# The last stage's products of a fused attention and two-layer MLP chain: seven block products for eight

## The reference, cut to what matters

```
attn_out = linear attention with decay, x = [3072, 512]
x = mixture of 8 experts over x (top 1), again [3072, 512]
a = x @ w1            # [3072, 1024]
b = x @ w2            # [3072, 1024]
out = ((a * b) @ w3) @ w_out     # [3072, 512]
```

## Time and profile before

| | us |
|---|---|
| median of 3 runs | 878.25 |
| lowest and highest | 874.43, 881.44 |
| profiled execution | 881.25 |
| its span, first to last instruction | 879.5 |
| TensorE busy | 855.1 |
| VectorE busy | 283.7 |
| ScalarE busy | 236.2 |
| GpSimd busy | 89.5 |
| mean granted clock of TensorE | 0.987 |

### The profile page before, as it was taken

The page is one execution under the profiler, slowest core; times in us unless marked ns, Lnnn a source line. Parts: engine busy times, 40 slices in busy tenths (PEclk is TensorE's granted clock), DMA queues, the critical chain, the costliest instruction groups (busy, mean ns, idle before and its releaser), DMA issues.

```text
span 879.5 us, 14619 instructions
## 1 busy us (share of the span) xinstructions
PE 855.1 (97%) x5722; PEld 733.0 (83%) x5723; DVE 283.7 (32%) x493; ACT 236.2 (27%) x382; POOL 89.5 (10%) x111
## 2 busy tenths in 40 slices
PE   9999999998999999999987999999999999999995
PEld 8899888787999988888876888888888888888884
DVE  3577698521221432111414430230230220220210
ACT  1334433321222432121334331231221221221210
POOL 2222002210102020202000001001001001001001
PEclk9999999999999999999997999999999999999998
DMA  9999881432022042303045002002002001001000
GB/s 332 330 327 306 295 314 48 147 108 83 26 71 96 9 182 95 96 0 96 31 160 156 1 2 95 1 6 90 0 14 81 0 28 68 0 8 41 1 12 37
DMA packets 43093, 83.36 MB, mean 95 GB/s; under 512 B 7345, under 2 KB 7985, under 8 KB 43057
## 3 DMA queue, kind: packets, MB, share of 16 engines
q1 hardware_dynamic: 33376, 60.08, 20.0%
q0 software_dynamic: 4736, 14.72, 5.2%
q10 hardware_dynamic: 4946, 8.08, 2.5%
HBM read 62.64 MB, written 20.22 MB: 94 GB/s over the span
## 4 chain that ended last, share of the span: by engine, by line
PE 93%; DVE 3%; issue 2%; ACT 1%; ACTq 1%; POOL 0%; DVEq 0%
PE bank L400 46%; PE attn L400 33%; PE bank L831 3%; PE attn L858 3%; PE pair L843 3%; PE pair L936 1%; PE bank L870 1%; PE attn L849 1%; PE bank L808 1%; PE bank L1019 1%; DVE w3T L1089 0%; PE pair L815 0%; ACTq L355 0%; DVE wc L1164 0%; DVE we_p L1089 0%
## 5 line engine op out<-in xcount | busy, mean ns | idle before, releaser
L400 PE MATMUL bank<-yT,wab 128*128 128x512 f32 x1152 | 265.1, 392 | 3.4 <-issue 3.4
L400 PEld LDWEIGHTS bank<-yT,wab 128*128 128x128 f32 x1152 | 218.2, 190 | 49.2 <-issue 3.6
L400 PE MATMUL bank<-xT,we_p 128*128 128x512 f32 (+1 forms) x672 | 140.6, 370 | 4.9 <-issue 3.8
L400 PE MATMUL attn<-hT,we_p 128*128 128x512 f32 (+1 forms) x672 | 141.8, 368 | 0.0
L400 PEld LDWEIGHTS bank<-xT,we_p 128*128 128x128 f32 x672 | 123.3, 190 | 21.7 <-issue 6.2
L400 PEld LDWEIGHTS attn<-hT,we_p 128*128 128x128 f32 x672 | 121.3, 188 | 14.4
L400 PE MATMUL attn<-wc,gT 128*128 128x512 f32 x576 | 131.5, 389 | 0.0
L400 PEld LDWEIGHTS attn<-wc,gT 128*128 128x128 f32 x576 | 108.1, 188 | 22.5
L1390 DVE TENSOR_TENSOR g<-bank,acopy 128x512 f32<-128x512 f32 x48 | 33.2, 691 | 255.0 <-PE bank L400 255.0
L1335 DVE SCALAR_TENSOR_TENSOR hT<-bank,hT 128x512 fp32r<-128x512 f32 x56 | 38.7, 690 | 151.5 <-ACT hT L661 151.5
L587 ACT ACTIVATE gT<-g 128x512 fp32r<-128x512 f32 x48 | 30.3, 632 | 137.6 <-DVE g L1390 137.6
(11 more groups left out here) (168 smaller groups left out, 609.2 us busy)
## 6 DMA issues: line engine op xcount, KB each, us to landing
we_raw<-in_moe_w_dram SPq DMA_DIRECT2D x6, 2048.0 KB, 8.9
yT_sorted<-yout ACTq DMA_DIRECT2D x7, 1024.0 KB, 4.4
qkv<-in_q_t_dram SPq DMA_DIRECT2D x24, 256.0 KB, 3.6
qkv<-in_v_dram SPq DMA_DIRECT2D x24, 256.0 KB, 5.0
x_rows<-x_keep SPq DMA_DIRECT2D x24, 256.0 KB, 3.6
ytile<-yT_sorted SPq DMA_DIRECT2D x6, 1024.0 KB, 5.3
qkv<-in_k_t_dram SPq DMA_DIRECT2D x23, 256.0 KB, 4.7
qkv<-in_k_dram SPq DMA_DIRECT2D x20, 256.0 KB, 5.2
```

The costliest lines, as they stand in the source:

```text
L400: i = pe.matmul(out_, left(a), right(b), start=(first and n == 0), stop=(last and n == 2), **kw)
```

## The change

Two groups (a pair, NP = 3 pairs) are done at a time. With the inputs cut in two halves of 256, the weights of one tile are a 2x2 block matrix A (row 1 is w1's tile, row 2 w2's; a block is two chunks), and the y of the two groups is a 2x2 block matrix B (a column is a group). The four results, a and b of both groups, come from seven block products ("factors", six matmuls each) instead of eight. The sums of y (T1 to T4) are made on VectorE once a pair; the sums of weights (S1 to S4) on GpSimd for each tile and pair, anew. A tile of a pair is called a quad, n = 0 to 23. The weights are no longer kept: each quad loads its 512 KB (w_load, three DMAs on SP), in two buffers, and splits all seven factors' weights. They are laid out on the host so that a tile is contiguous. The sums of products are made by three factors that add into one bank of PSUM, copies of it on ScalarE (p_one, u_two, u_three) and four additions on VectorE (c11, c12, c21, c22). Factor 3 of a quad is issued in the next one (`third`), or behind the last quad of a pair. After eight quads TensorE makes eight output tiles. The stage is written out, with no loop.

```diff
+    B11, B21, B22, T1, T2, T4, T3 = range(7)
+    A22, A11, A12, S2, S1, S3, S4 = range(7)
+    FACTORS = {1: (A11, B11), 2: (A12, B21), 3: (S4, B22), 4: (A22, T4), 5: (S1, T1), 6: (S2, T2), 7: (S3, T3)}
+    Y_ORDER = (B11, B21, T2, T1, T4, T3, B22)
+    W_PARTS = (slice(0, 3), slice(3, 6), slice(6, 7))
...
+            def w_load(n):
+                f, i = n % KF, n % 2
+                if n >= 2:
+                    sp.wait_ge(s_q[4], n - 1)
+                sp.dma_start(w_raw[i][:, A11:A12 + 1, :, :].rearrange("p a c m -> p (a c) m"), wa[f, :, :, :]).then_inc(s_wr[i], 16)
+                sp.dma_start(a21[i][:, :, :], wb[f, :, 0:HF, :]).then_inc(s_wr[i], 16)
+                sp.dma_start(w_raw[i][:, A22, :, :], wb[f, :, HF:KD, :]).then_inc(s_wr[i], 16)
...
+            def w_sums(n):
...
+                pool.wait_ge(s_wr[i], 48 * (n // 2 + 1))
+                if n >= 2:
+                    pool.wait_ge(s_q[7], n - 1)
+                pool.tensor_tensor(raw(S1), a21[i][:, :, :], raw(A22), ALU.add).then_inc(s_ws, 1)
+                pool.tensor_tensor(raw(S3), raw(A11), a21[i][:, :, :], ALU.subtract).then_inc(s_ws, 1)
+                pool.wait_ge(s_ws, 4 * n + 1)
+                pool.tensor_tensor(raw(S2), raw(S1), raw(A11), ALU.subtract).then_inc(s_ws, 1)
+                if n >= 2:
+                    pool.wait_ge(s_q[3], n - 1)
+                pool.wait_ge(s_ws, 4 * n + 3)
+                pool.tensor_tensor(raw(S4), raw(A12), raw(S2), ALU.subtract).then_inc(s_ws, 1)
...
+            def quad(n):                       # ScalarE
+                more, behind = n + 1 < NQ, n % KF > 0
                 if more:
+                    w_hi(n + 1, 0)
+                p_one_copy(n)
+                if more:
+                    w_hi(n + 1, 1)
+                if behind:
+                    g_hi(n - 1, 0)
+                if more:
+                    w_hi(n + 1, 2)
+                u_two_copy(n)
+                if behind:
+                    g_hi(n - 1, 1)
+                u_three_copy(n)
...
+                for t in range(TP):
+                    o_copy(p * TP + t)
+                    if p + 1 < NP and t:
+                        y_hi(p + 1, t - 1)
...
+            def third(n):
+                pe.wait_ge(s_c22, n + 1)
+                factor(3, n, bank[6 + n % 2], first=False)
+
+            def quad(n):                       # TensorE
+                sums, shared = bank[n % 2], bank[6 + n % 2]
+                if n >= 2:
+                    pe.wait_ge(s_u3, n - 1)
+                factor(1, n, sums)
+                if n:
+                    pe.wait_ge(s_c11, n)
+                factor(2, n, bank[2])
+                if n % KF:
+                    third(n - 1)
+                pe.wait_ge(s_u1, n + 1)
+                factor(6, n, sums, first=False)
+                if n >= 2:
+                    pe.wait_ge(s_c12, n - 1)
+                factor(5, n, shared)
+                if n:
+                    pe.wait_ge(s_c21, n)
+                factor(4, n, bank[3])
+                pe.wait_ge(s_u2, n + 1)
+                factor(7, n, sums, first=False)
...
+            for p in range(NP):
+                for n in range(p * KF, (p + 1) * KF):
+                    quad(n)
+                third(n)
+                for n in range(p * TP, (p + 1) * TP):
+                    out_rows_of(n)
...
+            def bilinear_inputs(run):
+                dve.wait_ge(s_w2lo, run * (KF // 2) + KF // 2)
+                y_sum(0, T1)
+                y_lo(0, 0)
+                w_lo(0, 0)
+                y_sum(0, T2)
+                y_sum(0, T4)
+                y_sum(0, T3)
+                y_lo(0, 1)
+                y_lo(0, 2)
+                w_lo(0, 1)
+                y_lo(0, 3)
+                y_lo(0, 4)
+                y_lo(0, 5)
+                w_lo(0, 2)
...
+            def quad(n):                       # VectorE
+                more, behind = n + 1 < NQ, n % KF > 0
+                if behind:
+                    c22(n - 1)
+                    c21(n - 1)
+                    bilinear(n - 1, 0)
+                c11(n)
+                if behind:
+                    c12(n - 1)
+                    bilinear(n - 1, 1)
+                if n == 0:
+                    y_lo(0, 6)
                 if more:
+                    w_lo(n + 1, 0)
+                    w_lo(n + 1, 1)
+                if behind:
+                    g_lo(n - 1, 0)
+                if more:
+                    w_lo(n + 1, 2)
+                if behind:
+                    g_lo(n - 1, 1)
```

More of the change, by code:

```diff
@@ L749, in _ @@
             act.sem_inc(s_yst, 16)
[L750 to L764, removed]
@@ L787, in _, with u_two_copy, u_three_copy @@
[L787 to L791, removed]
+            total = each_window(act, window)
+            def u_two_copy(n):
+                act.wait_ge(s_q[6], n + 1)
+                if n:
+                    act.wait_ge(s_c12, n)
+                copy(u_two[:, :], bank[n % 2][:, :]).then_inc(s_u2, 1)
+            def u_three_copy(n):
+                act.wait_ge(s_q[7], n + 1)
+                if n:
+                    act.wait_ge(s_c21, n)
+                copy(u_three[:, :], bank[n % 2][:, :]).then_inc(s_u3, 1)
@@ L1030, in _ @@
             pe.wait_ge(s_wclo, KF)
-            def group(g, more):
-                start = isinstance(g, int) and g == 0
-                for f in range(KF):
[L1036 to L1060, removed]
+            def factor(m, n, dst, first=True, last=True):
+                w, y = FACTORS[m]
+                p, i = n // KF, n % 2
+                if n % KF == 0:
+                    pe.wait_ge(s_yTlo, p * 7 + Y_ORDER.index(y) + 1)
+                if m in (1, 6, 3):
+                    pe.wait_ge(s_walo, 3 * n + (1, 6, 3).index(m) + 1)
+                for c in range(HF):
+                    mm = product(pe, dst[:, :], lambda a: wst[i][a][:, w, c, :], lambda a: y_op(a, y)[:, c, :], first and c == 0, last and c == HF - 1,
+                                 skip_group_check=True)
+                mm.then_inc(s_q[m], 1)
@@ L1406, in _, with c11, c12 @@
-            group(0, True)
-            with dve.Fori(1, NG - 1) as g:
-                group(g, True)
-            group(NG - 1, False)
+            def c11(n):
+                dve.wait_ge(s_q[2], n + 1)
+                dve.wait_ge(s_u1, n + 1)
+                if n:
+                    dve.wait_ge(s_g, 2 * n - 1)
+                tt(a_sum[0][:, :], bank[2][:, :], p_one[:, :], ALU.add).then_inc(s_c11, 1)
+            def c12(n):
+                dve.wait_ge(s_q[3], n + 1)
+                dve.wait_ge(s_u2, n + 1)
+                if n:
+                    dve.wait_ge(s_g, 2 * n)
+                tt(a_sum[1][:, :], bank[6 + n % 2][:, :], u_two[:, :], ALU.add).then_inc(s_c12, 1)
@@ new lines, in _ @@
+            for p in range(NP):
+                for n in range(p * KF, (p + 1) * KF):
+                    quad(n)
+                c22(n)
+                c21(n)
+                bilinear(n, 0)
+                c12(n)
+                bilinear(n, 1)
+                g_lo(n, 0)
+                g_lo(n, 1)
+                if p + 1 < NP:
+                    for m in (T1, T2, T4, T3):
+                        y_sum(p + 1, m)
+                    for i in range(7):
+                        y_lo(p + 1, i)
```

317 lines of the change are left out of this document (218 added, 99 removed).

## The result

| | before | changed |
|---|---|---|
| median, us | 878.94 (4 runs) | 858.03 (4 runs, 855.45 to 859.05) |
| profiled execution | 881.25 | 857.94 |
| its span | 879.5 | 855.9 |
| last stage, first matmul to end of last | 394.8 | 372.9 |

The ratio is 0.9766 (95% interval 0.9742 to 0.979): 20.9 us less at the medians, where 22.9 and 855 us were forecast. The spans differ by 23.6 us. So it is not shown that the 1.6 is the change's.

A forecast was written before the change was run, and what follows sets the result against it. TensorE was taken to bound the kernel, busy 855.1 of 879.5 us. The terms -32.6 + 4.6 + 1.2 + 2.9 + 1.0 = -22.9 us gave 858.3 for the profiled execution, 855 us against the median, range 849 to 873.

The forecast's parts named there:

- Matmuls: Last stage on TensorE: 42 matmuls instead of 48 in each of 24 quads, 144 fewer at 226.7 ns, -32.6 us.
- Pair ends: After a pair's last factor 7, TensorE waits for u_three and c22: 1.54 us at each of three pairs, +4.6 us.
- Pair starts: ScalarE's output copy, y_hi and w_hi stand ahead of p_one, so F6 waits 0.6 us twice, +1.2 us.
- Start: Stage start, behind the loop's exit: waits of 0.9 us on u_two and 2.0 on w_lo, +2.9 us (0 to 6).
- Condition tests: One more condition test per window on ScalarE behind the store of y: 3 x 0.3 us, +1.0 us (0 to 3).
- Body of the quad: Work beside TensorE within a quad hides behind its own 9.52 us of matmuls: cost 0.
- L: Landing time of a quad's 512 KB of weights: 3.5 us assumed, up to 3.7 free, then 2.2 us per 0.1 us.
- (a): Weights land late, delaying ScalarE's w_hi ahead of p_one: 881 us at L = 4.9, 895 at 5.5; in full, chance 0.07.
- (b): GpSimd and VectorE take turns, VectorE becomes the bound: 875 us; chance 0.16 together with a small part of late weights.
- (c): Each TensorE pause, three pair ends and the start, lets the clock fall at 3 us each: 867 us; chance 0.11.
- (d): Everything hides, the stage's start too, leaving -32.6 + 4.6: 850 us; chance 0.04 with better.

The follow-up runs named there:

- experiment 1: Kernel before with the fourth chunk of a left out in every group and tile, 144 matmuls fewer, nothing else moved: 846.17 us, ratio 0.9629.
- experiments 3 and 11: Changed kernel with a pair's last factor 3 issued inside the first output tile and g_lo moved ahead of the second product, run twice: 851.70 and 851.99 us.
- the second profile: The changed kernel itself, unedited, run again on another chip: 857.47 us, ratio 0.9734 to the kernel before.
- experiment 7: Changed kernel with GpSimd's four sums of weights replaced by fills with zero, which read nothing: 858.50 us, ratio 0.9762.
- Experiment 4: Changed kernel with each quad's weights loaded one factor later, after factor 7 instead of factor 4 of the quad two before: 882.22 us, ratio 1.0039.
- experiments 8 and 12: Changed kernel with factor 3 inside the output tile, quad 1's first weights made before the loop's exit, and y_hi moved, run twice: 847.27 and 847.64 us.
- experiment 5: Changed kernel with each of GpSimd's four sums of weights made twice in every quad: 893.09 us, ratio 1.017.

## Why the prediction was right, term by term

- **Matmuls, -32.6**: 32.6 in experiment 1. Right.
- **Pair ends, +4.6**: 4.4 of waits and 0.5 of restarts. Right; the chain of the earlier trace rows, 1.54 us, has the same links as this one of 1.47. Removing it (experiments 3 and 11) gives 5 to 6 us.
- **Pair starts, +1.2**: two waits of 0.23 us with restarts of 0.16, 0.8 in all. Right in place, a little too dear. A late load, which the sum had not, adds 0.5 in this profile.
- **Start, +2.9**: 2.8 here, 2.0 in the second profile, each with a restart. The mechanism of its larger part is shown by the chain, which runs through VectorE's exit from the loop to w_lo; the row of idle time ahead of c11 has 2.6 us for that exit, where 3.35 was borrowed from TensorE. The size is luck. The sum had 0.9 us on u_two, of which nothing came, and 2.0 on w_lo with low clock to 481 us; with low clock as long as that the wait is 1.2 to 1.3 (the table above). Here low clock ended at 476.5, so the wait was 2.8, and a second low stretch (486.8 to 490.2) followed. Low clock cost the stage about 3 us before and after, no term of the difference.
- **Condition tests, +1.0**: not seen; its 0.3 us a test was an estimate that no row bore out. The waits called "issue" are 6.0 us, 7.2 before.
- **Body of the quad, 0**: 49.63 of 50.00 us. Right for TensorE. Left out were small gaps, 9 to 12 restarts of under 0.2 us with no wait in the list, about 1.2 us together, and now and then weights that come late (a wait of 0.4 to 0.7 us each).

In the changed kernel's first profile: 359.1 of matmuls, 8.0 of waits (4.4 + 2.8 + 0.8), 1.1 of restarts at seven of them, 1.2 of small gaps, 3.1 for low clock: 372.5, against 372.9 measured.

Without the condition tests the sum had -23.9 us for the stage, and the stage gave -22.0; the small gaps and the late load are the difference. That the profiled execution came at 857.94, where the sum had 858.3, is partly luck: the stage's start lay 1.6 us earlier, which no term had. One number among the rivals does not follow from its price: at 2.2 us for each 0.1 us of L, 1% slower than before is reached at L = 5.15, not 5.3.

Two prices of covered work were off, and did no harm. GpSimd's sum of 256 columns was to take 0.55 us, half of one of 512; it takes 0.74 alone, 1.20 beside a VectorE instruction with two SBUF inputs here, and up to 1.77 in this profile:

```profile
518.58 0.74 POOL L635 TENSOR_TENSOR w_raw<-a,w_raw 128x256 f32<-128x256 f32 x1 [5.76 <-DMA w_raw<-in_moe_w_dram]
519.27 1.20 POOL L636 TENSOR_TENSOR w_raw<-w_raw,a 128x256 f32<-128x256 f32 x1
```

And the meeting goes both ways: VectorE's first product began at 518.75, behind GpSimd's sum, and took 1.12 us instead of 0.69. The one meeting of the earlier trace rows had shown only GpSimd waiting. The Trainium skill, SBUF — State Buffer, "Who interferes with whom", says that the order of issue decides which of the two is blocked, and that a VectorE instruction with two SBUF inputs contends with GpSimd instructions that read SBUF and not with those that only write it. The trace agrees in both directions; experiment 7, where GpSimd only writes and the product is back at 693 ns, agrees with the limit to reads.

**The rivals.** (a), late weights, was the near one: L came out at 3.2 to 4.4 us against 3.5 assumed. Its limit was too strict: 3.7 was allowed, and by the quad above (3.23 with 0.8 to spare) it is 4.0, which fits the wait of 0.37 at 4.39. Experiment 4 shows what 1.36 us more would have done, 24 us, with the price per quad that the rival had. (b) fell: the meetings are there, and its sign of sums over 1.0 us too, but VectorE has room for them (experiment 7). (c) fell at the pair ends, where the clock is 1.00 behind all three; its fourth pause, at the start, was followed by 0.50 in the first profile. (In the kernel before the clock fell at 460.8 us, behind the pause of 2.1 us but ahead of the one of 1.0, so the latter was no evidence for it.) (d) has 850 with the pair ends paid; experiments 8 and 12 come to 847.5, by moving those pauses, which it did not foresee.

## What to carry to other kernels

Where one engine is busy all the time, a removed instruction is worth its distance, and a scheme's real price is each place where that engine has no other work queued while a result goes round the others: count those, and give them other work (here three moved factors were worth 5 us). For covered work, read the slack from many periods and take the slow ones: a slack of 0.8 us in one quad was 0.4 in most, and 1.4 us less of it cost the whole gain. An engine's busy share says nothing of this; its place in another engine's order does.

## What the runs showed of the hardware

- The landing of 512 KB in three loads, with little else moving, took 3.2 to 4.4 us from the first issue to the reader's start, and 5.4 and 5.5 us in two quads of experiment 4. In the later of these the DMA moved 185 GB/s at 535 to 536 us and 2 and 5 GB/s in the two microseconds behind, and the reader started at 538.11; nothing in the profile explains it.
- A pause of TensorE costs 0.16 us beyond the wait that is listed.
- Pauses of 1.5 to 2.3 us inside the stage left the granted clock at 1.00. Of six pauses of 2.7 to 2.9 us, four were followed by 0.50 within 1.2 us (ahead of quad 1 in the changed kernel and in experiment 7, at 503.56 in experiment 4, at 620.41 in experiment 5) and two were not (2.73 us at 539.49 in experiment 4, 2.94 us at 755.82 in experiment 5).
- Leaving the loop with five turns unused took TensorE 3.4 us and VectorE 2.6 us.
